# Second products of the second expert layer as three float32r products of rounded parts and rests

## The reference

```python
def _moe2_ref(x, w_skip, w_gate, w1, w2):          # x: 1536 x 512, 8 experts, F = 1024
    do_compute = x @ w_skip > 0
    xc = x[do_compute]
    ...
    e_idx = np.argmax(xc @ w_gate, axis=1)
    ...
    for e in range(E):
        mask = e_idx == e
        ...
        h = np.maximum(xc[mask] @ w1[e], 0.0)
        y[mask] = gate_w[mask, None] * (h @ w2[e])
    out[do_compute] = xc + y
```

## Time and profile before

| | us |
|---|---|
| median of 3 runs | 630.75 |
| lowest and highest | 629.92, 631.79 |
| the profiled execution's own time | 632.04 |
| its span, first to last instruction | 630.0 |
| TensorE busy in the span | 607.7 (96%) |
| VectorE busy | 360.2 (57%) |
| ScalarE busy | 292.7 (46%) |
| POOL busy | 147.3 (23%) |

### The profile page before, as it was taken

How to read it: one execution, slowest core, us unless ns; L and a number is a source line. 1 busy time by engine, 2 the same in 40 slices (tenths; PEclk the granted TensorE clock), 3 DMA queues, 4 the chain that set the end, 5 groups by cost and what they waited for, 6 DMA issues and landing times.

```text
span 630.0 us, 11469 instructions
## 1 busy us (share of the span) xinstructions
PE 607.7 (96%) x4384; PEld 474.2 (75%) x4384; DVE 360.2 (57%) x1132; ACT 292.7 (46%) x525; POOL 147.3 (23%) x153
## 2 busy tenths in 40 slices
PE   7899999999999999888999999999999889999997
PEld 4667777767766765478898989899999867777774
DVE  5877776776776777787787878696502220000000
ACT  4877787777777678243534525251212201111111
POOL 6440303132133904101010101011333123333201
PEclk8999999999999999999999999999999999999999
DMA  7938936546473100644343627364896869999970
GB/s 176 239 84 187 216 90 152 126 110 162 106 217 67 32 4 2 232 161 160 134 166 128 227 85 269 121 230 150 269 324 242 303 214 335 351 344 352 332 271 20
DMA packets 73393, 116.38 MB, mean 185 GB/s; under 512 B 33799, under 2 KB 37161, under 8 KB 73058
## 3 DMA queue, kind: packets, MB, share of 16 engines
q1 hardware_dynamic: 68738, 106.75, 55.2%
q0 software_dynamic: 4016, 8.80, 4.0%
q10 hardware_dynamic: 576, 0.01, 0.0%
HBM read 87.76 MB, written 12.23 MB: 159 GB/s over the span
## 4 chain that ended last, share of the span: by engine, by line
PE 83%; DVE 6%; DMA 6%; issue 2%; ACT 2%; POOL 0%; SPq 0%; POOLq 0%; DVEq 0%
PE psB L1070 13%; PE psB L1084 11%; PE psB L356 10%; PE psB L1816 8%; PE psB L1831 8%; PE psA L326 6%; PE psB L341 6%; PE psA L328 5%; DMA xg<-x_scratch,recs 2%; PE psB L371 2%; DVE mx L477 2%; PE psA L1006 2%; DMA x_scratch<-x 1%; PE psB L1107 1%; PE psB L284 1%
## 5 line engine op out<-in xcount | busy, mean ns | idle before, releaser
L477 DVE TENSOR_REDUCE mx<-psA 128x1 f32<-128x768 f32 x96 | 91.6, 954 | 43.9 <-PE psA L328 43.1
L545 ACT ACTIVATE prob<-psA,ebi,esc 128x768 f32<-128x768 f32 x96 | 95.3, 992 | 31.9 <-DVE ebi L422 31.5
L1070 PE MATMUL psB<-xgT,w 128*128 128x192 f32 x512 | 91.9, 332 | 0.3 <-ACT xgT L1170 0.3
L1084 PE MATMUL psB<-hT,w 128*128 128x192 f32 x512 | 88.2, 330 | 0.0
L1070 PEld LDWEIGHTS psB<-xgT,w 128*128 128x128 f32 x512 | 82.5, 190 | 7.4 <-issue 3.6
L1084 PEld LDWEIGHTS psB<-hT,w 128*128 128x128 f32 x512 | 82.7, 190 | 0.3
L326 PE MATMUL psA<-kH,qT 128*128 128x384 f32 x192 | 73.8, 385 | 3.6 <-ACT prob L545 2.2
L1907 DVE SCALAR_TENSOR_TENSOR ob<-psB,recs,xg 128x512 f32<-128x512 f32 (+1 forms) x9 | 6.5, 721 | 108.7 <-PE psB L1831 101.3
L356 PE MATMUL psB<-pT,v_in 128*64 128x384 f32 x360 | 68.0, 499 | 0.0
L341 PE MATMUL psB<-identity_words,prob_words 128*128 128x128 f32 x576 | 64.4, 249 | 0.8 <-DVE pT L490 0.4
L328 PE MATMUL psA<-kB,qB 128*128 128x384 f32 x192 | 64.8, 337 | 0.0
(11 more groups left out here) (290 smaller groups left out, 849.7 us busy)
## 6 DMA issues: line engine op xcount, KB each, us to landing
w<-in_moe_w SPq DMA_DIRECT2D x34, 2048.0 KB, 9.7
kH<-hi SPq DMA_DIRECT2D x30, 192.0 KB
q_in<-in_q SPq DMA_DIRECT2D x16, 192.0 KB, 4.2
k_in<-in_k SPq DMA_DIRECT2D x16, 192.0 KB, 4.3
v_in<-in_v SPq DMA_DIRECT2D x8, 384.0 KB, 3.9
x_scratch<-x_of_batch SPq DMA_DIRECT2D x2, 1536.0 KB, 6.9
x_scratch<-x SPq DMA_DIRECT2D x8, 384.0 KB, 10.7
qT<-hi SPq DMA_DIRECT2D x15, 192.0 KB
```

The lines of the kernel that those rows point to most:

```text
L477: nc.vector.tensor_reduce(mx[:, u:u + 1], psS[u % 2][:, :, 0:HALF], AX.XY, ALU.max).then_inc(s_dv, 1)
L545: nc.scalar.activation(prob[:, u % 2, :, :], psS[u % 2][:, :, 0:HALF], ACT.Exp, bias=ebi[:, u:u + 1], scale=esc[:, u:u + 1], accum_out=den ...
L1070: ins = nc.tensor.matmul(ps[:, (f % 2) * CAP:(f % 2 + 1) * CAP], w1[:, k % 2, d, f * P:(f + 1) * P], xgT[:, k % 2, d, :], start=d == 0, st ...
L1084: ins = nc.tensor.matmul(ps[:, (d % 2) * CAP:(d % 2 + 1) * CAP], w2[:, k % 2, f, d * P:(d + 1) * P], hT[:, k % 2, f, :], start=f == 0, sto ...
```

## The change

For tiles 1 to 7 each of the eight second products is replaced by three float32r products: rounded hidden values times rounded weights, rounded hidden values times the weights' rests, and rests of the hidden values times rounded weights. float32r is a 32-bit format of TensorE with fewer digits; an operand has to be written as float32r by the engine that makes it. `words` gives a tile a second name of that type at the same place.

- ScalarE writes the rounded weights, `w2H`, in eight pieces of 128x512, four before each half of the rectified values. `w2H` has one buffer, so the pieces of tile t wait until the second product of tile t - 1 is done (`s_y`), and for the load of `w2`. The rectified values are written as float32r, which rounds them.
- VectorE writes the weights' rests, `w2` less `w2H`, over `w2` itself, each after its rounded piece, and the hidden rests `hL` in two halves from PSUM and the rounded values (`low`). All this stands in its queue ahead of the tile's `add`.
- TensorE waits for the weights' rests piece by piece (`s_wl`), for the hidden rests by half (`s_hl`), and for the hidden rests of the tile before ahead of a new first product, since they are read from `psH`.
- `w2H`, `hL` and an unused filler take the place of four tiles that only the routing uses. Tile 0 and the half tiles keep their float32 products.

```diff
@@ -112,6 +112,13 @@
 TD = 2
 
 NPLACED0, NPLACED = 4, 20
+
+
+def words(nc, sb, name, shape):
+
+    with nc.sbuf_tensor(name, shape, F32) as t:
+        pass
+    return t, sb(name + "_words", shape, F32R)
 
 
 def attention(nc, ctx, io, sb, sem, K):
@@ -834,17 +841,21 @@
     mcum = sb("mcum", [P, NJ + 1], BF16)
     left = sb("left", [P, NJ], F32)
     sl = sb("sl", [P, NJ], F32)
-    hit = sb("hit", [P, NJ, HT + P], F16)
     mark = sb("mark", [P, E], F32)
     Oa = sb("Oa", [P, NJ, E], BF16)
-    GB = sb("GB", [P, 4, N], BF16)
-    Gs = sb("Gs", [P, N], BF16)
-    cT = sb("cT", [P, N], F16)
+
+
+    with ExitStack() as routing_only:
+        GB, Gs, cT, hit = (routing_only.enter_context(nc.sbuf_tensor(n, shape, dt)) for n, shape, dt in (
+            ("GB", [P, 4, N], BF16), ("Gs", [P, N], BF16), ("cT", [P, N], F16), ("hit", [P, NJ, HT + P], F16)))
+    K["w2H"] = sb("w2_high", [P, KF, DM], F32R)
+    K["hL"] = sb("hT_low", [P, KF, P], F32R)
+    sb("routing_rest", [P, 832], F32)
 
     NX = 4
     xg, yT = K["xg"], K["yT"]
     xgT = sb("xgT", [P, 2, KD, CAP], F32)
-    hT = sb("hT", [P, 2, KF, CAP], F32)
+    hT, K["hTR"] = words(nc, sb, "hT", [P, 2, KF, CAP])
     x1 = sb("x1", [HT, NI, DM], F32)
 
     lgT = sb("lgT", [P, CAP], F32)
@@ -1616,6 +1627,12 @@
     xT = xgT[:, :, :, 0:P]
     hh = hT[:, :, :, 0:P]
 
+    hH, hL, w2H, w2L = K["hTR"][:, :, :, 0:P], K["hL"], K["w2H"], K["w2R"]
+    s_wh, s_wl, s_hl = sem("w2_high"), sem("w2_low"), sem("t_low")
+
+    def split(t):
+        return 1 <= t < E
+
     def tile_count(eng):
         eng.wait_ge(K["s_tab"], 1)
         return eng.value_load(tabi[0:1, 2 * NT2:2 * NT2 + 1], min_val=0, max_val=NT2)
@@ -1793,6 +1810,8 @@
 
                 for q in range(2):
                     pe.wait_ge(s_hr, 2 * (t - 1) + q + 1)
+                    if split(t - 1):
+                        pe.wait_ge(s_hl, 2 * (t - 2) + q + 1)
                     for k in range(KD):
                         for n, r in enumerate(HALVES):
                             at = n * DM + q * DH
@@ -1827,6 +1848,14 @@
             for f in range(first, last):
                 if f % 4 == 0:
                     pe.wait_ge(s_hr, 2 * t + f // 4 + 1)
+                if split(t):
+                    if f % 4 == 0:
+                        pe.wait_ge(s_hl, 2 * (t - 1) + f // 4 + 1)
+                    pe.wait_ge(s_wl, KF * (t - 1) + f + 1)
+                    nc.tensor.matmul(psY[t % 2][:, :], hH[:, t % 2, f, :], w2H[:, f, :], start=f == 0, stop=False)
+                    nc.tensor.matmul(psY[t % 2][:, :], hH[:, t % 2, f, :], w2L[:, k2 % 2, f, :], start=False, stop=False)
+                    ins = nc.tensor.matmul(psY[t % 2][:, :], hL[:, f, :], w2H[:, f, :], start=False, stop=f == KF - 1)
+                    continue
                 if t < E:
                     ins = nc.tensor.matmul(psY[t % 2][:, :], hh[:, t % 2, f, :], w2[:, k2 % 2, f, :],
                                            start=f == 0, stop=f == KF - 1)
@@ -1888,14 +1917,37 @@
                                    psU[:, q, 0:2 * P].rearrange("p (c r n) -> p c r n", c=2, r=2)).then_inc(s_hr, 1)
                 return
             for q in range(2):
+                if split(t):
+                    for f in range(4 * q, 4 * q + 4):
+                        if f == 0:
+                            act.wait_ge(s_w2[(E + t) % 2], 16 * ((E + t) // 2 + 1))
+                            if t > 1:
+                                act.wait_ge(s_y, t)
+                        nc.scalar.copy(w2H[:, f, :], w2[:, (E + t) % 2, f, :]).then_inc(s_wh, 1)
                 act.wait_ge(s_h, 2 * t + q + 1)
-                nc.scalar.activation(hh[:, t % 2, 4 * q:4 * q + 4, :],
+                to = hH if split(t) else hh
+                nc.scalar.activation(to[:, t % 2, 4 * q:4 * q + 4, :],
                                      psH[q][:, :].rearrange("p (f n) -> p f n", f=4), ACT.Relu).then_inc(s_hr, 1)
 
         tiles(act, copy, nothing, before=relu)
 
     def vector(dve):
+        def low(t):
+            for q in range(2):
+                for f in range(4 * q, 4 * q + 4):
+                    dve.wait_ge(s_wh, KF * (t - 1) + f + 1)
+                    w = w2[:, (E + t) % 2, f, :]
+                    nc.vector.tensor_tensor(w2L[:, (E + t) % 2, f, :], w, w2H[:, f, :].bitcast(F32), ALU.subtract
+                                            ).then_inc(s_wl, 1)
+                dve.wait_ge(s_hr, 2 * t + q + 1)
+                nc.vector.scalar_tensor_tensor(out=hL[:, 4 * q:4 * q + 4, :],
+                                               in0=psH[q][:, :].rearrange("p (f n) -> p f n", f=4), scalar=0.0,
+                                               in1=hH[:, t % 2, 4 * q:4 * q + 4, :].bitcast(F32), op0=ALU.max,
+                                               op1=ALU.subtract).then_inc(s_hl, 1)
+
         def add(t):
+            if split(t):
+                low(t)
             dve.wait_ge(s_y, t + 1)
             if t == 0:
                 dve.wait_ge(s_g[0], 16)
@@ -1977,7 +2029,7 @@
         K["xg"] = sb("xg", [P, 4, DM], F32)
         K["yT"] = sb("yT", [P, 2, KD, CAP], F32)
         K["w1"] = sb("w1", [P, 2, KD, F], F32)
-        K["w2"] = sb("w2", [P, 2, KF, DM], F32)
+        K["w2"], K["w2R"] = words(nc, sb, "w2", [P, 2, KF, DM])
 
         m_tensor, m_scalar, m_vector, m_pool, m_sync = middle(nc, io, sb, sem, K, link)
         g_vector, g_scalar, g_tensor, g_pool, g_table, g_totals = regroup(nc, io, sb, sem, K, link)
```

## The result

The changed kernel takes 621.21 us (median of four, 620.09 to 621.47) where the one before takes 630.42 (median of four); the ratio is 0.983, 95% interval 0.981 to 0.986. I had forecast 619.0 within 617.8 to 624.0. The gain is 9.2 us instead of 11.8: inside the range, but outside the 618 to 620.5 to which I gave the chance of 0.72.

A forecast was written before the change was run, and what follows sets the result against it. TensorE was taken to bound the kernel. Seven tiles saving 1.69 us each on the second product give 11.8 us off 630.75, all else costing nothing: 618.95, said as 619.0, range 617.8 to 624.0.

The forecast's parts named there:

- The bound: Tiles 1 to 7: TensorE never stops, 14.45 us from tile to tile, so a cheaper second product is saved whole.
- The price of a float32r product: Second product, 512 columns: 0.216 us each, 24 a tile 5.18 us, saving 1.69 us a tile, 11.8 in seven.
- Rival (a): Second product: each float32r product costs 0.228 us, so 9.7 us saved and a time of 621.0; chance 0.10.
- The added work: Per tile 6.7 us on ScalarE and 7.8 us on VectorE, ready before TensorE needs it; cost nothing.
- the cover: A tile's first products on TensorE, 7.14 us, during which ScalarE's and VectorE's new operations were to run unseen.
- Transposes: Between tiles: the next tile's transposed copy is still ready in time, with 0.5 us of slack; cost nothing.
- The transfers: Second weights are wanted earlier, by ScalarE; a late landing costs nothing or about 1 us, taken as nothing.
- rival (b): Transfers become the bound: 626 at 350 GB/s, about 620 at 375; chance 0.10 that it costs 2 us or more.
- The ceiling that I tried, 375 GB/s: If transfers stop at 375 GB/s, a tile's need 13.4 us, 0.7 more than TensorE.
- rival (c): VectorE and POOL exclude each other in tiles 1 to 5, TensorE waits 3.1 us a tile: 636; chance 0.05.
- the fifth product: TensorE reaches this second product 9.73 us into a tile; VectorE's last hidden rest, at 8.85, is ready by 0.9.

The follow-up runs named there:

- The products by themselves: Changed kernel plus ten rows of products run by TensorE behind its last product, other engines and transfers at rest; 652.36 us (one run).
- the engines' work alone: Changed kernel with both products with rests left out and the remaining one float32 in two passes; 631.72 us, ratio 1.000 to the kernel before.
- the doubled rests: Changed kernel with VectorE making each weight rest twice, once into a spare tile; 651.04 us (one run) beside 632.92 for the kernel before.
- the two repeats: The changed kernel timed again without edit in two calls; 623.57 us (ratio 0.986) and 620.95 us (ratio 0.984).
- one product of three: Changed kernel with both products with rests left out, ScalarE and VectorE still doing all their work; 614.04 us (two runs), ratio 0.972.

## Why the prediction was right, and where it was off

**The bound.** Right. TensorE is the chain through all seven tiles, before and after, and what it saves is saved.

**The price of a float32r product.** This is the term that was mis-sized: 24 x 0.216 = 5.18 us were forecast, 5.51 came, 0.33 us a tile and 2.3 us in all of the 2.6 that are missing. Rival (a) was the true case, to which I gave 0.10: I priced it at 621.0 and the median is 621.2. Its price was on paper and nearly exact; what was wrong was to give 0.72 to the other. The step that failed is the sentence by which I set its 0.015 us aside. I saw in the earlier trace rows that each weight load takes 0.19 us, longer than the 0.160 of streaming 384 columns, and took it for the cause; at 512 columns the load would be hidden. The products by themselves refute it: with half the columns of weights, whose load takes 0.13 us, nothing changes, and 512 columns carry 0.015 too. The rows of the same type, though of another width, were the better neighbours than rows of the same width and another type.

**The added work.** Right that it costs nothing: the engines' work alone gives a ratio of 1.000, and the doubled rests show that the cover is real and has an end. That the last rest ends 9.0 us into the tile for a forecast 8.85 is in part luck, for two errors cancel. I had the last four rests of the weights end at 8.1, behind the rectified copy, and release the hidden rest. They end at 7.5 (546.45 + 2.49); the rectified copy starts at 7.7, where I had 7.34, and it is this copy that the hidden rest waits for. I had added up durations, where I had gone by distances for TensorE: four rests of 0.69 us in a row take 2.49 and four casts of 0.62 take 2.18, since one starts before the other has ended. So the rests of the weights could have ended 0.8 us later before they touched that sum, and another 0.9 before TensorE had waited.

**Transposes.** Right: the first products of the next tile follow the last second product without a gap.

**The transfers, rival (b).** At nothing, as forecast, but nearer than its cost shows. One cast of the 56 waited for a load, and none in the two repeats; the view of waits in the changed kernel:

```profile
ACT w_high L1926 <- PE psB L1857: 4.3, 5, 0.9
...
ACT w_high L1926 <- DMA w<-in_moe_w: 1.3, 1, 1.3
```

That cast began at 555.24, 13.6 us after the load's issue at 541.64, where the earlier trace rows have 11.8 at most. The ceiling that I tried, 375 GB/s, was no ceiling but about what a tile of 13.1 us asks for (375 to 393 GB/s in tiles 2 to 6); 401 GB/s held for 47.5 us. By the figure of about 358 GB/s from HBM to one core, in "SBUF — State Buffer" of the Trainium skill, section "A bandwidth-pool intuition that's wrong (but worth ruling out)", the time would have been an estimated 624 us. Here the measurement decides: with one core at work it is not a cap, and it binds no tile.

**POOL and VectorE, rival (c).** The mechanism exists in one direction only. VectorE's rests took 0.68 to 0.715 us, with POOL's indirect transfers beside them, so VectorE hardly waited; POOL did, 0.3 us for a store, and nobody waits for that. The rule of the Trainium skill, "SBUF — State Buffer", section "SBUF: two separate sides", has the two exclude each other when VectorE has two SBUF inputs and GpSimd reads SBUF; the trace agrees in that POOL's transfer is held, and shows no case of the reverse. The loss that it would have made, through the fifth product, is what the doubled rests measured.

**Before tile 1.** Not in my sum. The start of tile 1 wanders by 5 us between executions, more than the error of the forecast; the median of four smooths it in part. 9.56 us is the gain of the tiles, 9.2 the difference of the medians. That they agree so well, and that 621.2 falls so near to the 621.0 of rival (a), owes something to luck: the same kernel had a median of 623.57 in another call.

## What to carry to other kernels

When an operation isn't in the trace at the size wanted, price it first from the same data type at another size, and keep its overhead unless a row shows it going away; an explanation for leaving it out is no such row. When the bound engine is freed, work out for each helper when its last piece is due and when it will be ready: this gave 9.0 against 9.9 us here, and a run that takes the cover away shows whether that is the true chain. Price a row of operations by the distance from start to start on every engine, not only on TensorE. Compare a repeated stretch (tile to tile) in the trace when the rest of the kernel moves by more than the effect.

## What the runs showed of the hardware

A float32r product is one pass, but costs 0.012 to 0.015 us more than its columns at 2.4 GHz, for 256 to 512 columns, with the same weights or others, alone or beside busy engines, each with its load of weights; a bf16 product of 512 columns costs 0.003 more. At 128 columns a float32r product costs 0.111 us, 0.058 more than its columns. Three float32r products of 512 columns (0.69 us) replace one float32 product (two passes, 0.86 us) for a gain of a fifth.

The transfers held 401 GB/s over 47.5 us at a DMA share of 1.04; before the change a tile's mean was 350 GB/s at 0.95, and that was demand, not capacity.

With the rests made twice, a wait of 2.9 us in a TensorE that is otherwise always busy was followed in three tiles of seven by products at the 1.2 GHz level (granted clock 0.52 in the 3.2 us behind one of them), and in the others by none; that cost 1.4 us in two tiles, where the clock was back at 1.00 before the tile ended, and 2.8 in the last. With one product of three it happened once, behind waits of 1.8 and 1.7 us: 0.53 from 584.8 to 588.9 us. A stall can cost more than its length. What decides between the two wasn't studied.

On VectorE and ScalarE operations in a row overlap: four rests of 0.69 us took 2.49 together, four casts of 0.62 took 2.18.

A faster variant is suggested but was not tried: the two products that hold a rest could take bf16 operands, 0.012 us less for each of 112, some 1.3 us in all, if the accuracy allows it and ScalarE's further casts find room. At 12 to 13 us a tile the transfers end such savings: casts already wait for loads in tiles of 12.76 us, and with one product of three the mean was 12.2.
